# Row sums' constant on GpSimd, reordered first loads, and later weight casts in the head of a window-attention and two-stage MLP kernel

## The chip, the cores and the metric

The kernel runs on one core of one Trainium2 chip. The metric is the device time of one execution in microseconds (us), the median of the runs. A core has five engines that run their own instruction streams and meet only at semaphores: TensorE (PE; its weight loads, PEld, overlap its matmuls), VectorE (DVE), ScalarE (ACT), GpSimd (POOL) and SyncE (SP), which here issues all DMAs. On-chip data lie in SBUF (128 partitions); matmul results land in PSUM banks.

## The reference, cut to what matters

```python
def _attn_ref(q, k, v):            # B=2, H=8, S=576, D=64, window 64
    scores = (1 / np.sqrt(D)) * np.matmul(q, k.transpose(0, 1, 3, 2))
    scores = np.where((rel >= 0) & (rel < window), scores, -1000000000.0)
    scores = scores - np.max(scores, axis=-1, keepdims=True)
    attn = np.exp(scores)
    attn = attn / (np.sum(attn, axis=-1, keepdims=True) + 1e-09)
    return np.matmul(attn, v)
...
    x = attention output as (1152, 512)
    h = x @ w_in; g = np.maximum(h, 0) + np.log1p(np.exp(-np.abs(h)))   # d_ff 2048
    x = g @ w_out
    p = domain_probs / (domain_probs.sum(-1, keepdims=True) + 1e-09)     # 4 experts, 1024 wide
    for e in range(4):
        out += p[:, e:e + 1] * (np.maximum(x @ w1[e], 0) @ w2[e])
```

## The kernel before, in words

Every float32 matmul of the two MLP stages is made of three matmuls on "high" and "low" parts: the high part is the value cast to the engine's rounded float32 type, the low part is what the cast lost. So each weight block is loaded raw, cast (high), and then subtracted (low).

The attention is cut into 24 units of 3 windows of 64 tokens for a pair of heads. Two units share one load of 1 MB (queries and keys, then values), called group 0 to 11. A unit u passes through these steps:

- `scores` on TensorE (line 986), three matmuls into one PSUM bank (`score_bank`); the last raises `score_done`.
- `masked_scores` on VectorE (line 665), mask and row maximum per window.
- `softmax_exp` on ScalarE (line 480), exponential with the row sum of each window; it raises `exp_done`.
- `row_inverse` on VectorE: line 674 adds the reference's 1e-9 (`EPS`) to the 128x3 row sums, and line 676 takes the reciprocal.
- `normalise_first` on VectorE (line 681, three `tensor_scalar`, one per window) for units 0 to 10; later units are normalised on GpSimd by `normalise` (line 422). Both raise `norm_done`.
- `transpose_probs` on TensorE (line 999), `copy_pT` on ScalarE (line 489), `weigh_values` on TensorE (line 1012), then `x_high` on ScalarE (line 496) and `x_low` on VectorE (line 689), which leave the input of the first MLP.

Units 0 to 9 are started ahead of the MLP. From then on a loop over steps k = 0, 1, ... does one 128-wide block of the first MLP a step: the up matmuls (line 1025), then softplus: on ScalarE `absolute` (504), `exponential` (509), `hidden_high` of the step before (521), `logarithm` (516); on VectorE `rounded` (697), `hidden_low` of the step before (716), `relu_ln` (703), `activation` (711); on GpSimd `lost` (429), on which `activation` waits. The down matmuls (1045) come three steps later. The remaining attention units are woven into the same steps: unit k + 10 is scored and exponentiated in step k, unit k + 8 is transposed and weighed. In every step each engine's order is fixed by the order of the calls; an engine waits at the first instruction whose semaphore isn't there, and everything behind it waits too.

The first weight blocks f = 0 to 4 are cast on VectorE (`up_high`, line 847) after the units that `FIRST_SPLIT` names: `{3: 0, 4: 1, 5: 2, 6: 3, 9: 4}`, that is, block 0 after unit 3 and so on. GpSimd subtracts their low parts in halves (`up_low_half`, line 433), ten halves i = 0 to 9. Halves 0 to 3 wait for the cast number i + 1; halves 4 to 9 wait until `norm_done` shows units 7, 8, 8, 9, 9, 9, which keeps them behind VectorE's normalisations. Ahead of half 8 come two halves of the first down block (`down_low_half`, line 440). Only then does GpSimd come to `lost` of step 0.

SyncE issues the loads in the written order on one queue: unit 0's queries and keys in two pieces, those of group 1, values of group 0 and 1, group 2, up weights pair 0, group 3, up weights pair 1, groups 4, 5, 6 (5 and 6 wait for slots), down weights pair 0, up weights pair 2 (which waits for the low parts of blocks 0 and 1, because it overwrites them), the gate's input `probs`, and more.

Of the kernel before, what the change touches and what calls it, by code (L numbers as in the profile page):

```python
# [10 lines left out]
P = 128  # L11
# [43 lines left out]
def two_stage_mlp_after_window_attention(nc, units, w_in, w_out, probs, w1, w2, out):  # L55
    ctx = ExitStack()
    with ctx:
# [152 lines left out]
        def score_bank(u):  # L210
            return ps_score[u % 2 if u < ALT_SCORED else 0]

        def pT_bank(u):
            return ps[3] if u < ALT_UNITS and u % 2 else ps_pT

# [32 lines left out]
        consts = sem("consts")  # L248
        score_done = sem("score_done")
        negmax_done = sem("negmax_done")  # L250
        first_maxima = sem("first_maxima")
        exp_done = sem("exp_done")
        eps_done = sem("eps_done")
        rinv_done = sem("rinv_done")
        norm_done = sem("norm_done")
        pT_done = sem("pT_done")
# [33 lines left out]

        FIRST_SPLIT = {3: 0, 4: 1, 5: 2, 6: 3, 9: 4}
        LATE_SPLIT = {1: 5, 3: 6, 4: 7}

        def f32(ap):
# [12 lines left out]
        def _(sp):  # L309
# [37 lines left out]
            sp.dma_start(slots[0][:, UNIT_QK:2 * UNIT_QK], units[0][:, UNIT_QK:2 * UNIT_QK]).then_inc(scores_landed[0], 16)  # L347
            first_queries_keys(1)
            first_values(0)
            first_values(1)  # L350
            attention_inputs(2)
            up_weights(0, up_in(0), (0,))
            attention_inputs(3)
            up_weights(0, up_in(0), (1,))
            attention_inputs(4)
            attention_inputs(5)
            attention_inputs(6)
            down_weights(0, down_in(0), (0,))
            up_weights(0, up_in(0), (2,))
            sp.dma_start(gate[:, :, :], probs.rearrange("(t p) e -> p t e", p=P)).then_inc(gate_in, 16)  # L360
            down_weights(0, down_in(0), (1,))
            attention_inputs(7)
            up_weights(0, up_in(0), (3,))
# [31 lines left out]
        @block.gpsimd  # L395
        def _(pool):
            steps = [0]

            def step(ins):

                steps[0] += 1
                ins.then_inc(consts, 1)
                pool.wait_ge(consts, steps[0])

            step(pool.memset(mask[:, :, :], 0.0))
            step(pool.memset(ident[:, :], 0.0))

            for h in range(2):
                m = mask[WIN * h:WIN * h + WIN, :, :]
                step(pool.affine_select(out=m, in_=m, compare_op=ALU.is_gt, fill=NEG, base=0,  # L410
                                        pattern=[[0, 2], [1, P]], channel_multiplier=-1))
                step(pool.affine_select(out=m, in_=m, compare_op=ALU.is_ge, fill=NEG, base=WIN,
                                        pattern=[[0, 2], [-1, P]], channel_multiplier=1))
            step(pool.memset(mask[:, 0, 0:WIN], NEG))
            step(pool.affine_select(out=ident[:, :], in_=ident[:, :], compare_op=ALU.not_equal, fill=1.0, base=0,
                                    pattern=[[-1, P]], channel_multiplier=1))
            assert steps[0] == N_CONSTS

            def normalise(u):
                pool.wait_ge(rinv_done, u + 1)  # L420
                p = prob[:, u % 3, :, :]
                pool.tensor_tensor(p, p, rinv[:, u % 3, :].rearrange("p (w o) -> p w o", o=1).to_broadcast([P, 3, P]),
                                   ALU.mult).then_inc(norm_done, 1)

            def lost(n, f):

                s, i = f % 2, h_count(n, f)
                pool.wait_ge(rnd_done, i)
                pool.tensor_tensor(sp_c[:, s, :], sp_e[:, s, :], sp_c[:, s, :], ALU.subtract).then_inc(lost_done, 1)  # L429

            def up_low_half(f, half):
                ks = slice(2 * half, 2 * half + 2)
                low = pool.tensor_tensor(wa[1][:, f, ks, :], raw_a[:, f // 2 % 2, ks, P * (f % 2):P * (f % 2) + P],
                                         f32(wa[0][:, f, ks, :]), ALU.subtract)
                if half == 1:
                    low.then_inc(wa_lo, 1)

            def down_low_half(half):
                cols = slice(DM // 2 * half, DM // 2 * half + DM // 2)
                low = pool.tensor_tensor(wb[1][:, 0, cols], raw_b[:, 0, 0, cols], f32(wb[0][:, 0, cols]), ALU.subtract)  # L440
                if half == 1:
                    low.then_inc(wb_lo, 1)

            for i in range(len(FIRST_SPLIT) - 1):
                pool.wait_ge(wa_hi, i + 1)
                up_low_half(i // 2, i % 2)
            for i, unit in zip(range(len(FIRST_SPLIT) - 1, 2 * len(FIRST_SPLIT)), (7, 8, 8, 9, 9, 9)):
                pool.wait_ge(norm_done, unit + 1)
                if i == 8:
                    pool.wait_ge(wb_hi, 1)  # L450
                    down_low_half(0)
                    down_low_half(1)
                    pool.wait_ge(wa_hi, 5)
                up_low_half(i // 2, i % 2)
            for k in range(STEPS):
                lost(k // FT, k % FT)
                if 0 < k < N_UNITS - SCORED:
                    normalise(k + SCORED)
# [186 lines left out]
        def _(dve):  # L645
# [9 lines left out]

            def masked_scores(u):

                dve.wait_ge(score_done, u + 1)
                if u >= 3:
                    dve.wait_ge(pT_done, u - 2)  # L660
                c, half, _ = unit_place(u)
                first = (2 * c + half) % 3 == 0
                for w in range(3):
                    m = 0 if first and w == 0 else 1
                    e = dve.tensor_tensor_reduce(prob[:, u % 3, w, :], score_bank(u)[:, P * w:P * w + P],
                                                 mask[:, m, :], -SCALE, BIG, ALU.add, ALU.min,
                                                 negmax[:, u % 3, w:w + 1])
                    if u == 0 and w < 2:
                        e.then_inc(first_maxima, 1)
                e.then_inc(negmax_done, 1)  # L670

            def row_inverse(u):
                dve.wait_ge(exp_done, u + 1)
                dve.tensor_scalar(rowsum[:, u % 3, :], rowsum[:, u % 3, :], EPS, None, ALU.add).then_inc(eps_done, 1)
                dve.wait_ge(eps_done, u + 1)
                dve.reciprocal(rinv[:, u % 3, :], rowsum[:, u % 3, :]).then_inc(rinv_done, 1)

            def normalise_first(u):
                dve.wait_ge(rinv_done, u + 1)
                for w in range(3):  # L680
                    m = dve.tensor_scalar(prob[:, u % 3, w, :], prob[:, u % 3, w, :], rinv[:, u % 3, w:w + 1], None,  # L681
                                          ALU.mult)
                m.then_inc(norm_done, 1)

            def x_low(u):
                dve.wait_ge(x_hi, u + 1)
# [287 lines left out]
        def _(pe):  # L974
            def scores(u):
# [7 lines left out]
                if u >= 2:  # L983
                    pe.wait_ge(negmax_done, last_of_score_bank(u))
                for w in range(3):
                    m = pe.matmul(score_bank(u)[:, P * w:P * w + P], q_slots[s][:, u % 2, w, :],  # L986
                                  k_slots[s][:, u % 2, WIN * w:WIN * w + P], start=True, stop=True)
                m.then_inc(score_done, 1)

            def transpose_probs(u):  # L990
# [223 lines left out]
```

## Time and profile before

| | before |
|---|---|
| median of 3 runs | 632.71 us (632.67 to 633.68) |
| the profiled execution, device time | 633.16 us |
| its span in the profile | 631.4 us |
| TensorE busy | 621.4 us, 98% of the span, 3892 matmul instructions |
| VectorE / ScalarE / GpSimd busy | 388.2 / 276.5 / 86.9 us |
| granted TensorE clock | full in all 40 slices |
| DMA | 40.78 MB, mean 65 GB/s; over 400 GB/s for most of the first 25 us |

The profile is one execution recorded by the hardware profiler. Its page gives the busy time of each engine; the chain of waits follows the work back from the last instruction, at each step to what released it; the timeline lists the instructions of an engine in order with the idle time ahead of each and what ended it. Times of rows are in us from the start of the span. Of the 10 us in which TensorE is idle, 5.5 lie before 20.95 us, 1.7 between there and 38 us, and 2.7 in the last 31 us, where the last results are stored; there is next to none between. The change touches the part up to 38 us.

### The profile page before, as it was taken

What the parts mean: (1) busy time and instruction counts of PE and PEld (TensorE: products, weight loads), DVE (VectorE), ACT (ScalarE), POOL (GpSimd) and SP (SyncE); (2) the same over time, 40 slices, a digit from 0 to 9 for tenths busy, and PEclk for the clock granted to TensorE, in tenths of its full rate; (3) what the DMA queues carried; (4) which work ended last, traced back from release to release, by engine and by line L of the source; (5) the groups of instructions that cost most, each with busy time, mean ns of one, the idle gap of its engine ahead of it and who ended that gap; (6) DMA issues with size and microseconds to landing.
All of it is one profiled execution on the core that took longest, in us unless ns stands there. A gap on an engine that the chain in (4) does not pass through costs nothing.

```text
span 631.4 us, 10158 instructions
## 1 busy us (share of the span) xinstructions
PE 621.4 (98%) x3892; PEld 578.6 (92%) x3892; DVE 388.2 (61%) x869; ACT 276.5 (44%) x635; POOL 86.9 (14%) x85
## 2 busy tenths in 40 slices
PE   7989999999999999999999999999999999999998
PEld 6789999999999999998998998988988988988987
DVE  5887665568645588897267267277276276376342
ACT  5887755556544465552342342332332332432410
POOL 1453333333333332000000000000000000000000
PEclk9999999999999999999999999999999999999999
DMA  8905230033200010022103003003003004000012
GB/s 326 375 36 194 75 134 1 19 115 134 67 2 0 2 33 28 7 68 94 42 0 101 34 1 100 34 1 104 31 1 113 21 1 123 12 0 1 2 51 100
DMA packets 11728, 40.78 MB, mean 65 GB/s; under 512 B 2336, under 2 KB 2592, under 8 KB 10400
## 3 DMA queue, kind: packets, MB, share of 16 engines
q1 hardware_dynamic: 11680, 40.13, 18.0%
q8 instruction: 31, 0.51, 0.3%
q14 instruction: 17, 0.14, 0.1%
HBM read 37.77 MB, written 2.36 MB: 64 GB/s over the span
## 4 chain that ended last, share of the span: by engine, by line
PE 95%; DMA 2%; SPq 1%; ACT 1%; DVE 0%; issue 0%
PE banks L1100 31%; PE banks L1076 28%; PE banks L1025 16%; PE banks L1045 16%; DMA part<-in_units 2%; PE banks L986 2%; PE banks L1012 1%; PE banks L999 1%; PE banks L1092 0%; SPq L315 0%; SPq L331 0%; DVE prob L681 0%; ACT prob L480 0%; SPq L323 0%; ACT sp_e L509 0%
## 5 line engine op out<-in xcount | busy, mean ns | idle before, releaser
L1100 PE MATMUL banks<-wb_hi,ehid_hi 128*128 128x512 f32 x284 | 110.5, 389 | 0.0
L1100 PE MATMUL banks<-wb_lo,ehid_hi 128*128 128x512 f32 x284 | 110.5, 389 | 0.0
L1100 PE MATMUL banks<-wb_hi,ehid_lo 128*128 128x512 f32 x284 | 110.5, 389 | 0.0
L429 POOL TENSOR_TENSOR sp_c<-sp_e,sp_c 128x384 f32<-128x384 f32 x48 | 64.1, 1336 | 135.5 <-DVE sp_c L697 135.5
L839 DVE SCALAR_TENSOR_TENSOR part<-banks,gate,part 128x512 f32<-128x512 f32 x62 | 46.6, 751 | 54.0 <-PE banks L1100 54.0
L1076 PE MATMUL banks<-T_lo,aop_hi 128*128 128x288 f32 x256 | 75.6, 295 | 0.0
L1076 PE MATMUL banks<-T_hi,aop_lo 128*128 128x288 f32 x256 | 75.6, 295 | 0.0
L1076 PE MATMUL banks<-T_hi,aop_hi 128*128 128x288 f32 x256 | 75.3, 294 | 0.0
L1025 PE MATMUL banks<-xy_hi,wa_hi 128*128 128x384 f32 x192 | 66.2, 345 | 0.0
L1045 PE MATMUL banks<-hid_hi,wb_hi 128*128 128x384 f32 x192 | 65.8, 343 | 0.0
L1045 PE MATMUL banks<-hid_hi,wb_lo 128*128 128x384 f32 x192 | 64.3, 335 | 0.0
L1045 PE MATMUL banks<-hid_lo,wb_hi 128*128 128x384 f32 x192 | 64.3, 335 | 0.0
L1025 PE MATMUL banks<-xy_hi,wa_lo 128*128 128x384 f32 x192 | 64.2, 335 | 0.0
L1025 PE MATMUL banks<-xy_lo,wa_hi 128*128 128x384 f32 x192 | 64.2, 334 | 0.0
L1100 PEld LDWEIGHTS banks<-wb_hi,ehid_lo 128*128 128x128 f32 x284 | 53.3, 188 | 11.1
L1100 PEld LDWEIGHTS banks<-wb_hi,ehid_hi 128*128 128x128 f32 x284 | 53.3, 188 | 10.8
L1100 PEld LDWEIGHTS banks<-wb_lo,ehid_hi 128*128 128x128 f32 x284 | 53.3, 188 | 10.7
L504 ACT ACTIVATE sp_e<-banks 128x384 f32<-128x384 f32 x48 | 23.5, 490 | 76.0 <-PE banks L1025 76.0
L1076 PE MATMUL banks<-B_hi,aop_lo 128*128 128x288 f32 x192 | 56.7, 295 | 0.0
L1076 PE MATMUL banks<-B_lo,aop_hi 128*128 128x288 f32 x192 | 56.6, 295 | 0.0
L1076 PE MATMUL banks<-B_hi,aop_hi 128*128 128x288 f32 x192 | 56.4, 294 | 0.0
L552 ACT ACTIVATE kept<-banks 128x576 f32<-128x576 f32 x16 | 10.4, 650 | 90.9 <-PE banks L1076 90.9
(105 smaller groups left out, 1245.6 us busy)
## 6 DMA issues: line engine op xcount, KB each, us to landing
unit_in<-in_units SPq DMA_DIRECT2D x8, 1024.0 KB, 6.7
raw_a<-in_w SPq DMA_DIRECT2D x16, 512.0 KB, 3.3
raw_b<-in_w SPq DMA_DIRECT2D x16, 512.0 KB, 3.3
raw_a<-in_w_in SPq DMA_DIRECT2D x8, 512.0 KB, 5.3
raw_b<-in_w_out SPq DMA_DIRECT2D x8, 512.0 KB, 4.1
part<-in_units SPq DMA_DIRECT2D x2, 1024.0 KB, 13.4
out_dram<-part SPq DMA_DIRECT2D x8, 256.0 KB, 2.0
unit_in<-in_units SPq DMA_DIRECT2D x2, 384.0 KB, 7.2
```

Of the source, the lines that this page charges most:

```text
L429: pool.tensor_tensor(sp_c[:, s, :], sp_e[:, s, :], sp_c[:, s, :], ALU.subtract).then_inc(lost_done, 1)
L504: act.activation(sp_e[:, s, :], up_bank(i - 1)[:, 0:CH], ACT.Abs).then_inc(abs_done, 1)
L552: act.activation(kept[i][:, :, :], Z[i], ACT.Copy).then_inc(p1_copied, 1)
L839: dve.scalar_tensor_tensor(out=acc[:, T, :], in0=TOKEN_BANKS[T], scalar=gate[:, T, e:e + 1], in1=acc[:, T, :], op0=ALU.mult, op1=ALU.add). ...
L986: m = pe.matmul(score_bank(u)[:, P * w:P * w + P], q_slots[s][:, u % 2, w, :], k_slots[s][:, u % 2, WIN * w:WIN * w + P], start=True, stop ...
L999: m = pe.transpose(pT_bank(u)[:, P * w:P * w + P], prob[:, u % 3, w, :], ident[:, :])
L1012: m = pe.matmul(o_bank(u)[D * h:D * h + D, WIN * w:WIN * w + WIN], v_slots[s][:, w, c:c + D], probT[:, u % 2, w, WIN * h:WIN * h + WIN], s ...
L1025: m = pe.matmul(bank[:, 0:CH], wa[a][:, f, k, :], xy[x][:, c, k, :], start=(k == 0 and i == 0), stop=(k == KT - 1 and i == 2))
L1045: m = pe.matmul(sums[t][:, 0:CH], wb[a][:, f, P * t:P * t + P], hid[x][:, f, :], start=(f == 0 and i == 0), stop=(f == FT - 1 and i == 2))
L1076: m = pe.matmul(into[:, s, :], aop[a][:, i, row, k, :], bop[name][b][:, k, HC * s:HC * s + HC], start=(fresh and k == 0 and j == 0), stop= ...
L1100: m = pe.matmul(TOKEN_BANKS[T], ehid[x][:, i, P * T:P * T + P], wb[a][:, f, :], start=(i == 0 and j == 0), stop=(i == 3 and j == 2))
```

## The change

It makes five edits.

1. The load order: group 2 ahead of group 1's values, group 3 ahead of up weights pair 0. `probs` is laid out on the host so that each partition's 36 values are one run of 144 bytes instead of nine of 16.
2. The casts: block 0 after unit 4 instead of 3, and so on up to block 3 after unit 7; block 4 stays after unit 9.
3. For units 2 to 9 the addition of `EPS` moves from VectorE to GpSimd (`add_eps`): units 2, 3, 4 ahead of half 0, then one ahead of each of halves 0 to 3 (units 5 to 8), and that of unit 9 ahead of half 5. Each waits for `exp_done` of its unit.
4. `normalise_first` becomes one `tensor_tensor` of 128x384 against the broadcast reciprocals, for units 0 to 10.
5. The three score matmuls of unit 0 go to three banks, each with its own signal, so that the mask and maximum of a window start before the other two are done.

```diff
+        def score_block(u, w):
+            bank = (score_bank(0), ps[1], ps[2])[w] if u == 0 else score_bank(u)
+            return bank[:, P * w:P * w + P]
...
-        FIRST_SPLIT = {3: 0, 4: 1, 5: 2, 6: 3, 9: 4}
+        FIRST_SPLIT = {4: 0, 5: 1, 6: 2, 7: 3, 9: 4}
+        EPS_AHEAD = range(2, SCORED)
...
             first_values(0)
+            attention_inputs(2)
             first_values(1)
-            attention_inputs(2)
+            attention_inputs(3)
             up_weights(0, up_in(0), (0,))
-            attention_inputs(3)
             up_weights(0, up_in(0), (1,))
...
-            sp.dma_start(gate[:, :, :], probs.rearrange("(t p) e -> p t e", p=P)).then_inc(gate_in, 16)
+            sp.dma_start(gate[:, :, :], probs).then_inc(gate_in, 16)
...
+            def add_eps(u):
+                pool.wait_ge(exp_done, u + 1)
+                pool.tensor_scalar(rowsum[:, u % 3, :], rowsum[:, u % 3, :], EPS, None, ALU.add).then_inc(eps_ahead, 1)
+
+            add_eps(2)
+            add_eps(3)
+            add_eps(4)
             for i in range(len(FIRST_SPLIT) - 1):
+                add_eps(5 + i)
                 pool.wait_ge(wa_hi, i + 1)
                 up_low_half(i // 2, i % 2)
             for i, unit in zip(range(len(FIRST_SPLIT) - 1, 2 * len(FIRST_SPLIT)), (7, 8, 8, 9, 9, 9)):
+                if i == 5:
+                    add_eps(unit + 1)
                 pool.wait_ge(norm_done, unit + 1)
...
-                dve.wait_ge(score_done, u + 1)
+                if u > 0:
+                    dve.wait_ge(score_done, u + 1)
...
+                    if u == 0 and w < 2:
+                        dve.wait_ge(first_scores, w + 1)
+                    elif u == 0:
+                        dve.wait_ge(score_done, 1)
...
-                dve.tensor_scalar(rowsum[:, u % 3, :], rowsum[:, u % 3, :], EPS, None, ALU.add).then_inc(eps_done, 1)
-                dve.wait_ge(eps_done, u + 1)
+                if u not in EPS_AHEAD:
+                    dve.tensor_scalar(rowsum[:, u % 3, :], rowsum[:, u % 3, :], EPS, None,
+                                      ALU.add).then_inc(eps_done, 1)
+                if u in EPS_AHEAD:
+                    dve.wait_ge(eps_ahead, u - EPS_AHEAD[0] + 1)
+                else:
+                    dve.wait_ge(eps_done, u + 1 if u < EPS_AHEAD[0] else u + 1 - len(EPS_AHEAD))
                 dve.reciprocal(rinv[:, u % 3, :], rowsum[:, u % 3, :]).then_inc(rinv_done, 1)
...
-                for w in range(3):
-                    m = dve.tensor_scalar(prob[:, u % 3, w, :], prob[:, u % 3, w, :], rinv[:, u % 3, w:w + 1], None,
-                                          ALU.mult)
-                m.then_inc(norm_done, 1)
+                p = prob[:, u % 3, :, :]
+                dve.tensor_tensor(p, p, rinv[:, u % 3, :].rearrange("p (w o) -> p w o", o=1).to_broadcast([P, 3, P]),
+                                  ALU.mult).then_inc(norm_done, 1)
```

## Rows read from the trace of the kernel before

**Rows 1.** The page: busy time of TensorE, share of the span, instructions
```profile
PE 621.4 (98%) x3892; PEld 578.6 (92%) x3892; DVE 388.2 (61%) x869; ACT 276.5 (44%) x635; POOL 86.9 (14%) x85
```

**Rows 2.** Chain of waits, first 90 us: start, duration, what the end waited for
```profile
5.83 15.08 DMA part<-in_units
...
37.27 0.45 issue
```

**Rows 3.** Timeline of TensorE, first 40 us: start, duration, instruction, idle before
```profile
8.09 0.94 PE L986 MATMUL banks<-unit_in 128*128 128x128 f32 x6 [1.99 <-DMA unit_in<-in_units]
...
26.17 0.44 PE L1025 MATMUL banks<-xy_hi,wa_hi 128*128 128x384 f32 x1
...
33.97 0.55 PE L999 MATMUL banks<-ident,prob 128*128 128x128 f32 x3 [1.06 <-DVE prob L681]
```

**Rows 4.** Timeline of GpSimd, first 45 us
```profile
3.64 0.15 POOL L414 MEMSET mask<- 128x64 f32 x1
...
26.42 1.43 POOL L433 TENSOR_TENSOR wa_lo<-raw_a,wa_hi 128x256 fp32r<-128x256 f32 x2 [1.17 <-DVE prob L681]
28.96 0.84 POOL L433 TENSOR_TENSOR wa_lo<-raw_a,wa_hi 128x256 fp32r<-128x256 f32 x1 [1.12 <-DVE prob L681]
29.77 1.54 POOL L440 TENSOR_TENSOR wb_lo<-raw_b,wb_hi 128x256 fp32r<-128x256 f32 x2
31.27 1.41 POOL L433 TENSOR_TENSOR wa_lo<-raw_a,wa_hi 128x256 fp32r<-128x256 f32 x2
32.64 0.99 POOL L429 TENSOR_TENSOR sp_c<-sp_e,sp_c 128x384 f32<-128x384 f32 x1
...
37.22 1.07 POOL L422 TENSOR_TENSOR prob<-prob,rinv 128x384 f32<-128x384 f32 x1 [0.59 <-DVE rinv L676]
```

**Rows 5.** Timeline of VectorE, first 40 us
```profile
27.79 0.17 DVE L674 TENSOR_SCALAR rowsum<-rowsum 128x3 f32<-128x3 f32 x1 [0.79 <-ACT prob L480]
...
28.20 0.68 DVE L681 TENSOR_SCALAR prob<-prob,rinv 128x128 f32<-128x128 f32 x3
28.80 0.42 DVE L847 CAST wa_hi<-raw_a 128x512 fp32r<-128x512 f32 x1
29.56 0.29 DVE L665 CUSTOM_DVE_ANT_0 prob<-banks,mask 128x128 f32<-128x128 f32 x1 [0.34 <-PE banks L986]
...
30.20 0.52 DVE L697 TENSOR_SCALAR sp_c<-sp_e 128x384 f32<-128x384 f32 x1
...
32.31 1.60 DVE L681 TENSOR_SCALAR prob<-prob,rinv 128x128 f32<-128x128 f32 x3
33.83 0.55 DVE L711 TENSOR_TENSOR sp_l<-sp_l,sp_c 128x384 f32<-128x384 f32 x1
...
34.93 0.35 DVE L697 TENSOR_SCALAR sp_c<-sp_e 128x384 f32<-128x384 f32 x1
...
37.05 0.55 DVE L711 TENSOR_TENSOR sp_l<-sp_l,sp_c 128x384 f32<-128x384 f32 x1
37.51 1.32 DVE L648 TENSOR_TENSOR wa_lo<-raw_a,wa_hi 128x512 fp32r<-128x512 f32 x1
```

**Rows 6.** Instructions of line 648: count, then shortest, median and longest in ns
```profile
L648 DVE TENSOR_TENSOR wa_lo<-raw_a,wa_hi x11: 676/684/1319, 37.5 to 148.8; 128x512 fp32r<-128x512 f32 x11
```

**Rows 7.** Timeline of ScalarE, first 40 us
```profile
24.35 0.19 ACT L480 ACTIVATION_READ_ACCUMULATOR prob<-prob,negmax 128x1 f32 x1
...
27.57 0.19 ACT L480 ACTIVATION_READ_ACCUMULATOR prob<-prob,negmax 128x1 f32 x1
...
34.41 0.53 ACT L521 ACTIVATE hid_hi<-sp_l 128x384 fp32r<-128x384 f32 x1 [1.25 <-DVE sp_l L711]
...
37.14 0.47 ACT L489 ACTIVATE probT<-banks 128x384 f32<-128x384 f32 x1
```

**Rows 8.** SyncE's queue: the issue of up weights pair 2
```profile
23.45 0.33 SPq L331 DMA_DIRECT2D raw_a<-in_w_in  x1
```

**Rows 9.** Its time from issue to landing, us
```profile
DMA to landing us min/median/max: 4.9/4.9/4.9
```

More of the change, by code:

```diff
@@ L250, in two_stage_mlp_after_window_attention @@
         negmax_done = sem("negmax_done")
+        first_scores = sem("first_scores")
         first_maxima = sem("first_maxima")
@@ L253, in two_stage_mlp_after_window_attention @@
         eps_done = sem("eps_done")
+        eps_ahead = sem("eps_ahead")
         rinv_done = sem("rinv_done")
@@ L664, in masked_scores @@
                     m = 0 if first and w == 0 else 1
-                    e = dve.tensor_tensor_reduce(prob[:, u % 3, w, :], score_bank(u)[:, P * w:P * w + P],
+                    if u == 0 and w < 2:
+                        dve.wait_ge(first_scores, w + 1)
+                    elif u == 0:
+                        dve.wait_ge(score_done, 1)
+                    e = dve.tensor_tensor_reduce(prob[:, u % 3, w, :], score_block(u, w),
                                                  mask[:, m, :], -SCALE, BIG, ALU.add, ALU.min,
@@ L985, in scores @@
                 for w in range(3):
-                    m = pe.matmul(score_bank(u)[:, P * w:P * w + P], q_slots[s][:, u % 2, w, :],
+                    m = pe.matmul(score_block(u, w), q_slots[s][:, u % 2, w, :],
                                   k_slots[s][:, u % 2, WIN * w:WIN * w + P], start=True, stop=True)
+                    if u == 0 and w < 2:
+                        m.then_inc(first_scores, 1)
                 m.then_inc(score_done, 1)
@@ L1199 @@
         "w_out": inputs["moe_w_out"].reshape(FF1 // 256, 2, P, DM).transpose(0, 2, 1, 3),
-        "probs": inputs["moe2_domain_probs"],
+        "probs": inputs["moe2_domain_probs"].reshape(N_TOK, P, NE).transpose(1, 0, 2),
         "w1": np.stack([w1[:, 0, :, :, 0], w1[:, 1, :, :, 0], w1[:, 1, :, :, 1], w1[:, 0, :, :, 1]]).transpose(
```

## The prediction

> **What bounds the kernel now.** I read the page first: TensorE is busy 621.4 of 631.4 us [rows 1], so a change outside its work can only move the 10 us in which it idles. The chain of waits then shows where these lie. Its first long piece is the transfer of group 4, issued at 5.83 and landed 15.08 later, at 20.91 [rows 2]; the scores of unit 8 start on it at 20.95. Behind that the chain is TensorE with two real stalls: 1.06 us ahead of the transpose of unit 10 at 33.97 [rows 3], and 0.45 us ahead of the value matmuls of unit 10, W10 for short, which start at 37.27 + 0.45 = 37.72 [rows 2]. From W10 on the chain has no further gap up to 90 us. So two clocks count: when group 4 lands, and when W10 may start. Whatever the change does between is worth what it moves W10, and nothing more.
>
> What W10 waits for is read backwards. Its input is copied by ScalarE at 37.14 [rows 7]. ScalarE's order in step 1 is hidden_high, logarithm, x_high, exponentials of unit 11, a weight cast, then that copy; it runs through these without a pause from 34.41, where it had idled 1.25 us for VectorE's `activation` of step 0 [rows 7]. That one started at 33.83 [rows 5]. It needs two things: VectorE must be through the normalisation of unit 10 (three instructions, 32.31, 1.60 us) [rows 5], and GpSimd's `lost` of step 0 must be done: 32.64 + 0.99 = 33.63 [rows 4]. They came within 0.2 us of each other. So W10 starts 37.72 - 33.83 = 3.89 us after `activation`, and the change has to be judged by the later of these two.
>
> **Load order, gate, late casts: nothing, with cover.** The bytes ahead of group 4 are the same and it is still issued last of them, so I keep 20.91; groups 2 and 3 land earlier and the work behind them then waits longer for group 4. Bounds: if the order of packets changes how evenly the engines drain, some tenths of a us either way; I take 0. The first scores of unit 0 in three banks: the next thing TensorE does, scores of unit 2, waits for a transfer until 8.09, 1.99 us idle [rows 3], and an earlier softmax of unit 0 ends inside that wait. 0. The casts one unit later, and `add_eps` of unit 8 ahead of half 3, hold up the low part of block 1. That addition can't start before the exponentials of unit 8 end at 24.35 + 0.19 = 24.54 [rows 7]; add about 0.15 and a half of about 0.7, and the low part stands at 25.45. TensorE wants it at 26.17 [rows 3]: 0.7 us of cover. SyncE's load of up weights pair 2, which waited for the same low part and was issued at 23.45 [rows 8], moves to about 25.5, with the gate, down weights pair 1 and group 7 behind it. It landed 4.9 us after its issue [rows 9], behind a full queue; with the same 4.9 it lands at 30.4, with a shorter queue nearer 29. The cast that needs it comes at about 29.5 in the sum below, so it costs 0 to 0.9 us on VectorE, whose next steps have some slack. I take 0.
>
> **The transpose of unit 10: a gain that is not kept.** The three `tensor_scalar` of unit 10 took 1.60 us where unit 9's took 0.68 [rows 5], because the second lay under GpSimd's `lost`. One `tensor_tensor` of 384 columns takes 0.46 us to the next instruction (37.05 to 37.51) [rows 5]. Started at 32.31, or a little later, it lets the transpose run at about 32.9 to 33.4: 0.6 to 1.06 us earlier. But TensorE then only reaches W10's wait earlier.
>
> **GpSimd's `lost` of step 0: the term that decides.** Before, halves 5 and 6 ran at 26.42 to 27.85, in a time when GpSimd would otherwise wait, and half 7 began at 28.96, behind the normalisation of unit 9 [rows 4]. Now `add_eps` of unit 9 stands ahead of half 5, and waits for the exponentials of unit 9, which end at 27.57 + 0.19 = 27.76 [rows 7]; these hang on TensorE's order behind group 4 and don't move. Seven pieces (halves 5, 6, 7, two down halves, 8, 9) then stand between 27.76 and `lost`, instead of five from 28.96.
>
> 1. The addition: the trace has no such instruction on GpSimd. A memset of 64 columns took 0.15 [rows 4], a half of 256 columns 0.7; three columns lie nearest to the memset. With 0.08 us until GpSimd sees the signal (the normalisation ended at 28.88, half 7 began at 28.96 [rows 4, 5]) half 5 starts at about 27.95; bounds 27.8 and 28.5.
> 2. Seven pieces at 31.27 to 32.64 for two, 0.69 each [rows 4]: 4.83 us.
> 3. What VectorE takes from them. The rows show that the two engines don't run side by side in these operations. `split_up` of 512 columns took 1.32 us at 37.51, under GpSimd's normalisation 37.22 to 38.29 [rows 4, 5], where its median is 0.684 [rows 6]; so it began to work at 38.15, 0.14 before GpSimd's recorded end. `rounded` took 0.52 at 30.20 instead of 0.35 at 34.93 [rows 5], and the two down halves around it 1.54 instead of 1.41 [rows 4]: 0.13 for a `tensor_scalar` of 384 columns. Half 7 took 0.84 for 0.72 (1.43 for two at 26.42), its start lying 0.16 into the cast at 28.80 [rows 4, 5]: 0.12, and 0.2 if the two had met squarely. Four such meetings now lie in GpSimd's run: the normalisation of unit 9 (wanted at about 28.2, in the middle of half 5; a `tensor_tensor` with both inputs in SBUF, 0.46 less the 0.14 of overlap: 0.33), the cast of block 4 (behind half 6, 0.2), `rounded` (0.13 to 0.2), the normalisation of unit 10 (0.33). Sum 1.0; bounds 0 and the full lengths of the four, 0.46 + 0.33 + 0.27 + 0.46 = 1.5.
>
> `lost` then starts at 27.95 + 4.83 + 1.0 = 33.8, ends at 34.8, and `activation` starts at about 34.9 instead of 33.83: 1.1 later. ScalarE's row of step 1 follows at once, and W10 starts at 38.8. ScalarE's other waits in that row (maxima of unit 11) hang on the same VectorE order and move with it. TensorE has no idle time behind W10 from which to make this good.
>
> The Trainium skill ("SBUF — State Buffer", Who interferes with whom) says that VectorE with two SBUF inputs and GpSimd share a port pair by an exclusive lock: the one that issues first keeps it for the whole instruction. The trace agrees in kind (1.32 for 0.684 us) [rows 5, 6], but VectorE got in 0.14 us before the recorded end. Taken to the letter, the rule gives the upper bound of item 3.
>
> **The sum.** Span 631.4 + 1.1 = 632.5 us, device time of the profiled execution 633.16 + 1.1 = 634.3. That execution was 0.45 above the median of the runs, so against 632.71 I say 633.8 us, 0.17% longer. A difference under about 0.2%, 1.27 us, is what a measurement of this kernel can't tell from none. So the forecast is "same", close to its upper edge.
>
> **The rivals.**
> A. The forecast, W10 later by 0.8 to 1.4 us: 0.47, of which 0.13 over 1.27.
> B. VectorE and GpSimd hardly hinder each other here, because the `tensor_tensor` fits between GpSimd's accesses: only the late start of half 5 counts, 27.95 + 4.83 + 0.99 = 33.8 for the end of `lost`, W10 later by 0 to 0.8, time 632.7 to 633.5, middle 632.9. For it: `activation` at 37.05 kept its 0.55 although GpSimd began at 37.22 [rows 4, 5]. Against: GpSimd's instruction then took 1.07. 0.20.
> C. Slower: each meeting costs GpSimd the whole VectorE instruction, and after each both want the port at once. The place is 28.2 to 33.2; `lost` ends at 27.98 + 4.9 + 1.5 + 0.99 = 35.4, W10 is 1.6 later, 634.3. It decides from the point at which the four meetings cost over 1.2 us together, or the addition over 0.35 us instead of 0.15. With a small GpSimd instruction of 0.5 us it is 634.7. 0.24.
> D. Group 4 lands at another time, since the transfers ahead of it are reordered. For a result faster than 631.44 it must land 2.4 us earlier, or 1.3 if the rest stays as before. The same bytes stand ahead of it, issued by the same time, which speaks against. Earlier enough 0.05, later enough 0.04.
> That the change does what it is shaped for, all the 1.06 us of unit 10 kept, would need `lost` done by about 32.8; GpSimd alone forbids it (item 2 with nothing for item 3 already ends at 33.8), so it has no chance of its own.
>
> **How the numbers follow.** Faster is the early half of D: 0.05. Slower is 0.13 of A, C and the late part of D: 0.41. Same is the rest of A and B: 0.54. The range runs from inside B to C with a dearer addition: 632.5 to 635.0; outside remain D early and the ends of B and C, under 0.2.
>
> **What would show it.** In the changed profile: scores of unit 8 at 20.9 still, with some 1.5 us of idle ahead of it instead of a few tenths; half 5 at about 28.0, right behind a short addition; the normalisations of units 9 and 10 longer than 0.55 us; the transpose of unit 10 near 33.3; `lost` at 33.8; `activation` right behind its end; the wait ahead of W10 grown from 0.45 to about 2.2 us. The forecast is wrong if half 5 starts before 27.8, if `lost` starts before 33.2 or after 34.5, if ScalarE's hidden_high isn't released by `activation`, or if unit 8's scores leave 20.9 by more than 0.3.

## The result and the profile after

| | before | after |
|---|---|---|
| median | 632.89 us (632.67 to 633.68, 6 runs) | 635.84 us (634.64 to 636.99, 6 runs) |
| ratio | | 1.0046, 95% interval 1.0036 to 1.0056 |
| profiled execution, its span | 633.16, 631.4 us | 635.89, 634.1 us |
| mean granted TensorE clock | 1.00 | 0.997 (0.994 in two other runs) |

The change costs 2.95 us, 0.46%. The forecast was 633.8 us, 0.17%, with a range up to 635.0: too little. In the profiled executions all of the loss lies ahead of W10, the value matmuls of unit 10, as in the forecast: behind W10 both spans have 593.7 us left (631.4 - 37.72 and 634.1 - 40.43). Of all the executions below one, of b3 (682.5 us, mean clock 0.852), was over 1.5% above the fastest of its kernel; it counts in that run's median and in no ratio, share or other count.

TensorE's timeline after the change, first 45 us: start, duration, instruction, idle time before it. Line 1012 are scores, 1027 transposes, 1040 value matmuls.

```profile
7.69 0.94 PE L1012 MATMUL banks<-unit_in 128*128 128x128 f32 x6 [1.09 <-DMA unit_in<-in_units]
...
21.05 0.94 PE L1012 MATMUL banks<-part 128*128 128x128 f32 x6 [2.42 <-DMA part<-in_units]
...
23.85 1.48 PE L1012 MATMUL banks<-part 128*128 128x128 f32 x6
25.27 0.91 PE L1040 MATMUL banks<-probT,part 128*64 128x64 f32 x12
...
27.28 0.57 PE L1040 MATMUL banks<-probT,part 128*64 128x64 f32 x12
...
35.70 0.55 PE L1027 MATMUL banks<-ident,prob 128*128 128x128 f32 x3 [0.96 <-DVE prob L708]
...
40.43 0.57 PE L1040 MATMUL banks<-probT,unit_in 128*64 128x64 f32 x12 [1.41 <-issue]
```

The same groups before (line 986 are scores, 999 transposes, 1012 value matmuls):

```profile
20.02 0.55 PE L999 MATMUL banks<-ident,prob 128*128 128x128 f32 x3 [0.34 <-DVE prob L681]
20.95 0.94 PE L986 MATMUL banks<-part 128*128 128x128 f32 x6 [0.39 <-DMA part<-in_units]
...
25.67 0.57 PE L1012 MATMUL banks<-probT,part 128*64 128x64 f32 x12
...
37.72 0.57 PE L1012 MATMUL banks<-probT,unit_in 128*64 128x64 f32 x12 [0.45 <-issue]
```

Group 4 landed where it did (scores of unit 8 at 21.05, before 20.95), but TensorE had idled 2.42 us for it instead of 0.39. The scores of unit 9 then took 1.48 us and the value matmuls of unit 6 0.91, where such groups otherwise take 0.83 and 0.57. The windows say why. Columns: stretch, its length, busy time of TensorE, its weight loads, VectorE, ScalarE, GpSimd, then the granted clock, DMA share, GB/s:

```profile
18.65:21.05 2.40, 0.01 (x1) 0.01 (x1) 1.59 (x8) 1.64 (x7) 1.33 (x4) 1.00 0.99 396
21.05:22.50 1.45, 1.45 (x19) 1.26 (x20) 0.48 (x5) 0.00 (x0) 0.36 (x1) 1.00 1.00 412
22.50:26.00 3.50, 3.50 (x24) 3.26 (x24) 2.12 (x13) 1.97 (x8) 1.07 (x3) 0.53 0.74 303
26.00:28.00 2.00, 1.90 (x23) 1.44 (x20) 1.27 (x6) 0.94 (x3) 0.57 (x1) 0.98 0.44 147
```

Behind the idle stretch the granted clock is at half, the lower of its two levels (1.2 instead of 2.4 GHz), for 3.4 us (from 22.7 to 26.1); before the change it stayed at 1.00 here. TensorE is what everything hangs on in this stretch, so the slow clock goes straight into the time: from the scores of unit 8 to the value matmuls of unit 7 it is 27.28 - 21.05 = 6.23 us, before 25.67 - 20.95 = 4.72. That is 1.51 us. From there to W10 it is 13.15 us, before 12.05: 1.10 us. With 0.10 for the landing these make 2.71, the difference of the profiled executions (635.89 - 633.16 = 2.73).

The second term is the one that was forecast. GpSimd after the change (line 453 is `add_eps`, 440 and 447 the halves, 436 `lost`), to be read beside [rows 4]:

```profile
24.85 0.23 POOL L453 TENSOR_SCALAR rowsum<-rowsum 128x3 f32<-128x3 f32 x1 [3.44 <-ACT prob L497]
25.16 1.41 POOL L440 TENSOR_TENSOR wa_lo<-raw_a,wa_hi 128x256 fp32r<-128x256 f32 x2
29.45 0.23 POOL L453 TENSOR_SCALAR rowsum<-rowsum 128x3 f32<-128x3 f32 x1 [2.88 <-ACT prob L497]
29.75 2.61 POOL L440 TENSOR_TENSOR wa_lo<-raw_a,wa_hi 128x256 fp32r<-128x256 f32 x3
32.32 1.53 POOL L447 TENSOR_TENSOR wb_lo<-raw_b,wb_hi 128x256 fp32r<-128x256 f32 x2
33.82 1.41 POOL L440 TENSOR_TENSOR wa_lo<-raw_a,wa_hi 128x256 fp32r<-128x256 f32 x2
35.20 1.31 POOL L436 TENSOR_TENSOR sp_c<-sp_e,sp_c 128x384 f32<-128x384 f32 x1
```

And VectorE, to be read beside [rows 5] (708 normalisation, 873 cast, 723 `rounded`, 729 `relu_ln`, 697 the addition of unit 10, 737 `activation`):

```profile
29.99 0.91 DVE L708 TENSOR_TENSOR prob<-prob,rinv 128x384 f32<-128x384 f32 x1
30.82 0.95 DVE L873 CAST wa_hi<-raw_a 128x512 fp32r<-128x512 f32 x1
...
32.32 0.95 DVE L723 TENSOR_SCALAR sp_c<-sp_e 128x384 f32<-128x384 f32 x1
33.19 0.54 DVE L729 SCALAR_TENSOR_TENSOR sp_l<-banks,sp_l 128x384 f32<-128x384 f32 x1
...
33.92 0.65 DVE L697 TENSOR_SCALAR rowsum<-rowsum 128x3 f32<-128x3 f32 x1
...
34.82 0.83 DVE L708 TENSOR_TENSOR prob<-prob,rinv 128x384 f32<-128x384 f32 x1
36.54 0.56 DVE L737 TENSOR_TENSOR sp_l<-sp_l,sp_c 128x384 f32<-128x384 f32 x1 [0.89 <-POOL sp_c L436]
```

The addition on GpSimd waits 2.88 us for the exponentials of unit 9. Seven pieces follow without a pause. The normalisations, the cast, `rounded` and the small addition of unit 10 on VectorE, which meet them, take 1.5 to 4 times their time (0.91 and 0.83 for 0.56, 0.95 for 0.42, 0.95 for 0.35, 0.65 for 0.17). `relu_ln`, which reads PSUM, keeps its 0.54 (0.55 at 40.12 before). `activation` waits 0.89 us for `lost`, and W10 comes 40.43 - 36.54 = 3.89 us behind `activation`, exactly as before.

### The profile page after: what moved, and what is told of

It is laid out like the page before. It is cut to its first block, busy times and chain, and to the rows that moved or that the text cites. A ratio compares the mean times of both kernels' runs of the same rounds, so it can differ in the third digit from the quotient of the medians.

```text
span 634.1 us, 10144 instructions
## 1 busy us (share of the span) xinstructions
PE 623.3 (98%) x3892; PEld 580.5 (92%) x3892; DVE 387.4 (61%) x839; ACT 276.7 (44%) x635; POOL 89.3 (14%) x93
## 4 chain that ended last, share of the span: by engine, by line
PE 95%; DMA 2%; DVE 1%; SPq 1%; issue 1%; ACT 0%; POOL 0%; DVEq 0%
PE banks L1128 30%; PE banks L1104 28%; PE banks L1073 16%; PE banks L1053 16%; DMA part<-in_units 2%; PE banks L1012 2%; PE banks L1040 1%; PE banks L1027 1%; PE banks L1120 0%; ACT prob L497 0%; SPq L322 0%; SPq L338 0%; SPq L330 0%; DVE wa_hi L873 0%; DVE prob L708 0%
## 6 DMA issues: line engine op xcount, KB each, us to landing
part<-in_units SPq DMA_DIRECT2D x2, 1024.0 KB, 13.1
```

## The experiments

There are two suspects: the clock (TensorE idle ahead of group 4, 1.5 us) and GpSimd's `lost` (1.1 us). Since a single execution either has a stretch at half clock or not, each run is also read by how many of its executions have a mean granted clock of 0.997 or less. One half-clock stretch of 3.4 us makes 0.997 of 634 us, two make 0.995. After the change this was so in 6 of 6, and in the kernel before, in the runs beside the experiments, in 10 of 99.

The ratio is close to that of the mean times, so it gives a few long times more weight than the median does (a4 above all). The kernel before was run again beside each set: its medians were 632.96 us for the runs a, 632.89 for the runs b, 632.74 for the runs c.

| run | ratio to before | median us | executions with a clock of 0.997 or less |
|---|---|---|---|
| a1 fill | 1.0029 (1.0019 to 1.0038) | 634.74 | 4 of 10 |
| a2 unit 9 | 1.0005 (0.9989 to 1.0021) | 633.08 | 6 of 10 |
| a3 both | 1.0002 (0.9993 to 1.0012) | 633.19 | 0 of 10 |
| a4 old load order | 1.0024 (1.0004 to 1.0044) | 633.68 | 4 of 10 |
| c1 old load order, unit 9 | 0.9991 (0.9981 to 1.0000) | 632.20 | 1 of 10 |
| b1 loads and casts on before | 1.0009 (0.9999 to 1.0020) | 633.76 | 6 of 10 |
| b2 GpSimd late on before | 1.0019 (1.0010 to 1.0029) | 633.96 | 2 of 10 |
| c4 normalisation on before | 0.9998 (0.9989 to 1.0007) | 632.85 | 3 of 10 |
| b3 two fills, unit 9 | 0.9996 (0.9987 to 1.0005) | 633.11 | 0 of 9 |
| b4 `lost` first on before | 0.9990 (0.9981 to 0.9999) | 632.17 | 1 of 11 |
| c2 the same, blocks spread | 0.9980 (0.9971 to 0.9989) | 631.87 | 1 of 11 |
| c3 b3 and c2 together | 0.9986 (0.9977 to 0.9995) | 631.91 | 2 of 12 |

**a1, the idle stretch filled.** On the changed kernel:

```diff
+            for _ in range(8):
+                pe.matmul(ps[0][:, 0:P], warm[:, :], warm[:, :], start=True, stop=True)
             scores(UPC)
```

> The changed kernel with eight matmuls on the zeroed warm-up tile (results unused, bank ps[0]) between the transpose of unit 5 and the scores of unit 8, so that TensorE works through most of the 2.42 us in which it was idle. Theory 1 (clock: the idle stretch ahead of group 4's landing lets the granted clock fall to half from 22.5 to 26.1, worth 1.6 us; GpSimd's late lost of step 0 the other 1.1): granted clock 1.00 throughout, transpose of unit 7 at 24.5 to 24.7, W10 at 38.7 to 38.9, about 1.6 us under the changed kernel and 1.1 over the kernel before. Rival (the clock falls for a reason that isn't the idle stretch, as the chip's state): granted clock 0.5 there as before, time unchanged.

In the profiled execution the clock stayed at 1.00, and W10 came 38.30 - 20.33 = 17.97 us after the scores of unit 8, 1.2 over the 16.77 of before: the half-clock term is gone, the GpSimd term stands. The median fell by 1.1 us, not 1.6, because 4 of 10 executions still had a slow stretch (635.1 to 636.0 us); the six at full clock have a median of 633.97, 1.0 over before. None of the four has a profile, so the place of their stretch wasn't seen; a4 below suggests where.

**a2, the addition of unit 9 back on VectorE.**

```diff
-        EPS_AHEAD = range(2, SCORED)
+        EPS_AHEAD = range(2, SCORED - 1)
...
-                if i == 5:
-                    add_eps(unit + 1)
```

> The changed kernel with unit 9's addition back on VectorE, so that half 5 on GpSimd no longer waits for unit 9's exponentials. Theory 1: the clock still falls (idle 2.4 us ahead of unit 8's scores), halves 5 and 6 run right behind half 4, lost of step 0 starts 1.0 to 1.4 us earlier than the 35.20 of the changed kernel, W10 about 1.0 earlier, 1.6 to 1.9 us over the kernel before. Rival (GpSimd's order doesn't matter, all is the clock): lost moves but W10 doesn't, time as the changed kernel.

It gained more than expected, 2.8 us on the changed kernel's 635.84. In the profile W10 is 37.70 - 20.59 = 17.11 us after unit 8's scores, against 17.97 in a1, so the addition's place was worth 0.9. The rest is the spread of the clock: 6 of 10 executions have it under 1 (633.0 to 635.9 us), the four others lie at 631.8 to 632.0, under the kernel before. In this profile the half clock lies at another place, behind the wait for group 1. The windows of TensorE alone (length, busy time, granted clock, DMA share, GB/s):

```profile
6.50:8.60 2.10, 0.00 (x1) 1.00 1.03 421
8.60:12.10 3.50, 3.50 (x17) 0.53 1.02 425
12.10:14.00 1.90, 1.90 (x29) 0.97 0.98 410
```

There it cost nothing ahead of group 4, since TensorE still had to wait for it afterwards (0.20 us, until 20.59). So what a slow stretch costs depends on what comes behind it.

**a3, both edits.**

> Both edits together: filling matmuls and unit 9's addition on VectorE. Theory 1: both losses gone, within 0.4 us of the kernel before (the remaining difference is unit 10's transpose, earlier by 0.6 to 1.0, which ends in the wait of W10). If the two terms don't add up to all of the loss, it stays over 1 us above.

As expected: within 0.3 us of before, and no execution of ten with a slow clock, against 6 of 10 in a2, whose only difference is the eight matmuls. This pair, with b3 below (0 of 9), carries the claim that idle time is what lets the clock fall here. It doesn't say where: a2's one profiled fall lay behind the wait for group 1, which a3 leaves unfilled (1.03 us there in its profile). And the filling saved next to no time: a3's median of 633.19 us isn't under a2's 633.08. The filling was too long for the best executions: unit 8's scores began at 20.24 straight behind it, without a wait for the transfer.

**a4, the load order of before in the changed kernel.**

> The changed kernel with the load order of before (group 1's values ahead of group 2, up weights pair 0 ahead of group 3); casts, additions and normalisation as changed. Theory 1: groups 2 and 3 land about 1 us later, the idle stretch ahead of unit 8's scores shrinks to 1.0 to 1.5 us; if the clock then holds, 1.6 us under the changed kernel, if it still falls, the faster VectorE row is a cause beside the load order. Rival (the order of packets itself slows things): group 4 would land at another time than 20.9 to 21.0.

TensorE idled 1.50 us ahead of unit 8's scores (group 4 landed at 21.56 here), and the clock held there. It fell elsewhere, behind the wait ahead of W10:

```profile
39.54 0.57 PE L1040 MATMUL banks<-probT,unit_in 128*64 128x64 f32 x12 [2.13 <-issue]
```

```profile
37.40:39.54 2.14, 0.01 (x2) 1.00 0.00 0
39.54:40.10 0.56, 0.56 (x13) 0.99 0.00 0
40.10:43.40 3.30, 3.30 (x12) 0.50 0.00 0
43.40:45.00 1.60, 1.60 (x14) 0.97 0.00 0
```

(First fence: TensorE's timeline; second: its windows.) The landing at 21.56 is the sign that I gave for the rival, but the other profiles show landings as far apart with either load order (see rival D below), so it doesn't speak for it. The fall ahead of W10's row I had not foreseen: where the transpose of unit 10 comes early, GpSimd's lateness gathers in one long wait ahead of W10, and this can cost a slow stretch too, 1.5 us: 634.7 - 39.54 = 595.2 us are left behind W10 instead of 593.7. Five of the six executions at full clock took 632.7 to 632.9 us, no more than before, although GpSimd is as late here as in the changed kernel; more on that under c1.

**c1, the load order of before and unit 9's addition on VectorE.**

> The changed kernel with the load order of before and unit 9's addition on VectorE; the one difference from the run with the load order of before is that GpSimd's lost of step 0 comes earlier, so that TensorE idles about 1.4 instead of 2.13 us ahead of W10. Theory 1 (the half clock seen from 40 us in that run follows the long idle stretch ahead of W10): no fall behind W10, fewer executions with a clock under 1 than 4 of 10, median 632.0 to 632.6. Rival (falls come from the head alone): as many executions under 1.

1 of 10 executions with a slow clock instead of 4 of 10, and 632.20 us, 0.5 under the 632.74 of before beside it, with an interval that reaches 1. The profiled execution happened to be the one with a fall. It began 0.7 us behind the end of a stretch of 1.43 us idle ahead of unit 8, so a fall in the head doesn't need the new load order.

With a2 it separates the loads: the same kernel with the new load order has 6 of 10. Ten executions each are few, and all runs together are firmer: with the new load order and no filling 18 of 26 executions had a slow clock (after, a2, b1), with the old one 22 of 161 (before, a4, b2, b4, c1, c2, c4). The late casts are in 20 of the latter (a4, c1), with 5.

At full clock the rest of the change does gain. a2's four such executions (631.8 to 632.0 us) and c1's nine (632.1 to 632.8) are under before, and five of a4's six aren't above it in spite of GpSimd. No such execution of these three has a profile, so where they gain wasn't seen. A reading that fits, and isn't shown: TensorE is ready for group 4 earlier than before (end of unit 5's transpose at 18.6 us in the changed kernel, 19.3 in c1, 20.6 before), which is worth something whenever group 4 lands early.

**b1, load order and late casts alone, on the kernel before.** The edit is the two diffs of the change on `attention_inputs(2)`, `attention_inputs(3)` and `FIRST_SPLIT`.

> The kernel before with two parts of the change alone: groups 2 and 3 loaded ahead, and the casts of blocks 0 to 3 one unit later. Additions and normalisation stay on VectorE as before. Theory 1 (the clock falls where TensorE idles about 2 us): VectorE still holds unit 5 to 7 back, so the idle stretch ahead of unit 8's scores is 1 to 1.6 us; clock 1.00 in most executions, time within 0.5 us of before, W10 16.8 after unit 8's scores as before. Rival (the new load order is what makes executions spread): median over 1 us above before with clocks under 1.

The rival came nearer to the truth: 6 of 10 executions with a slow clock. In the profile the idle stretch ahead of unit 8's scores was 1.03 us, 0.34 us of idle lay a little ahead of it, and the clock fell 0.35 us after the scores had begun:

```profile
18.57 0.55 PE L999 MATMUL banks<-ident,prob 128*128 128x128 f32 x3 [0.34 <-DVE prob L681]
20.14 1.35 PE L986 MATMUL banks<-part 128*128 128x128 f32 x6 [1.03 <-DMA part<-in_units]
```

```profile
19.10:20.14 1.04, 0.01 (x1) 1.00 0.97 394
20.14:23.50 3.36, 3.35 (x23) 0.55 1.02 417
```

So the falls come without the moved additions and the single normalisation, and 2 us of idle time aren't needed. That it is the load order and not the late casts, which b1 has too, is said by a4 and c1 (5 of 20 with the casts late and the old order). W10 was 38.41 - 20.14 = 18.27 us after unit 8's scores, 1.50 over before, the price of one stretch once more.

**b2, GpSimd's halves 5 and 6 late, on the kernel before.**

```diff
-            for i, unit in zip(range(len(FIRST_SPLIT) - 1, 2 * len(FIRST_SPLIT)), (7, 8, 8, 9, 9, 9)):
+            for i, unit in zip(range(len(FIRST_SPLIT) - 1, 2 * len(FIRST_SPLIT)), (7, 9, 9, 9, 9, 9)):
```

> The kernel before with one edit: halves 5 and 6 on GpSimd wait for the normalisation of unit 9 instead of unit 8, so that seven pieces stand between 28.9 and lost of step 0, with no other part of the change. Theory 1: lost starts at 34.0 instead of 32.64, W10 1.2 to 1.4 later, time 1.2 to 1.4 us over before; transposes up to unit 10 where they were. If the idle stretch ahead of W10 reaches 2 us the clock may fall behind it in some executions, another 1.5. Rival (GpSimd's order has slack): time as before.

The executions with full clock lie at 633.7 to 634.7, their middle at 633.9, 1.0 over before (1.1 over its executions at full clock). The GpSimd term is thus shown alone, on the old kernel, with no other part of the change. The profiled execution is one of the two with a fall, which came 0.5 us after the scores of unit 8 had begun, with the old load order and an idle stretch of 1.07 us:

```profile
21.03 1.19 PE L986 MATMUL banks<-part 128*128 128x128 f32 x6 [1.07 <-DMA part<-in_units]
```

```profile
30.53 2.35 POOL L433 TENSOR_TENSOR wa_lo<-raw_a,wa_hi 128x256 fp32r<-128x256 f32 x3 [5.48 <-DVE prob L681]
32.84 1.42 POOL L440 TENSOR_TENSOR wb_lo<-raw_b,wb_hi 128x256 fp32r<-128x256 f32 x2
34.22 1.41 POOL L433 TENSOR_TENSOR wa_lo<-raw_a,wa_hi 128x256 fp32r<-128x256 f32 x2
35.58 1.01 POOL L429 TENSOR_TENSOR sp_c<-sp_e,sp_c 128x384 f32<-128x384 f32 x1
```

From the value matmuls of unit 7, behind the fall, to W10 it is 40.52 - 27.25 = 13.27 us, 1.2 over the 12.05 of before.

**c4, the normalisation by one instruction alone, on the kernel before.**

> The kernel before with the normalisation of units 0 to 10 by one tensor_tensor and nothing else of the change. Theory 1 (a gain that isn't kept): VectorE 0.13 us a unit faster up to unit 9, transpose of unit 10 at 33.2 to 33.4 instead of 33.97, but W10 where it was within 0.2 us, since lost of step 0 and ScalarE's row set it; time within 0.3 us of before; the idle stretch ahead of W10 grows from 0.45 to about 1.1. Rival: the transpose's 0.7 us is kept, time 0.6 us under before.

No gain, as expected, but for another reason than I gave. The transpose of unit 10 wasn't earlier at all (13.1 us after unit 8's scores, before 13.0), for the single instruction waited behind `lost` as the three had. VectorE (674 the addition, 681 the normalisation), then GpSimd:

```profile
31.72 0.75 DVE L674 TENSOR_SCALAR rowsum<-rowsum 128x3 f32<-128x3 f32 x1 [0.53 <-ACT prob L480]
32.50 0.18 DVE L676 RECIPROCAL rinv<-rowsum 128x3 f32<-128x3 f32 x1
32.71 1.10 DVE L681 TENSOR_TENSOR prob<-prob,rinv 128x384 f32<-128x384 f32 x1
```

```profile
32.39 1.00 POOL L429 TENSOR_TENSOR sp_c<-sp_e,sp_c 128x384 f32<-128x384 f32 x1
```

0.68 of the 1.10 us lie under `lost` (32.71 to 33.39). The idle stretch ahead of W10 didn't grow either (0.44 us instead of the 1.1 expected).

**b3, two shorter fills.** On a2: three filling matmuls ahead of `scores(2)`, four ahead of `scores(UPC)`, the scores of unit 8.

> The changed kernel with unit 9's addition on VectorE and filling matmuls in two places, three ahead of the scores of unit 2 and four ahead of those of unit 8 (results unused). Theory 1: neither idle stretch reaches 2 us, clock 1.00 in nearly all executions, and with only four instead of eight filling matmuls the scores of unit 8 start as soon as group 4 lands: median 632.0 to 632.8, spread under 1.5 us. Rival (clock falls without an idle stretch of that length): executions with a clock under 1 stay as many as without the fills (6 of 10).

No execution of nine had a slow clock (one at 0.999). The median (633.08 of these nine) missed the expectation by 0.3: the executions fall into two lots, 631.8 to 632.2 and 633.1 to 633.8, between which the clock doesn't differ. In the profiled one, of the lower lot, group 4's scores start at 19.71. I take the landing of group 4 to be the cause, but the upper lot has no profile, so this stays open.

**b4 and c2, `lost` ahead of the last halves, on the kernel before.** c2 in full (b4 has `{2: 5, 3: 6, 4: 7}`):

```diff
-        LATE_SPLIT = {1: 5, 3: 6, 4: 7}
+        LATE_SPLIT = {2: 5, 4: 6, 5: 7}
...
                     down_low_half(1)
+                    lost(0, 0)
+                    pool.wait_ge(norm_done, SCORED + 1)
                     pool.wait_ge(wa_hi, 5)
...
-                lost(k // FT, k % FT)
+                if k > 0:
+                    lost(k // FT, k % FT)
...
             def normalise_first(u):
                 dve.wait_ge(rinv_done, u + 1)
+                if u == SCORED:
+                    p = prob[:, u % 3, :, :]
+                    dve.tensor_tensor(p, p, rinv[:, u % 3, :].rearrange("p (w o) -> p w o", o=1).to_broadcast([P, 3, P]),
+                                      ALU.mult).then_inc(norm_done, 1)
+                    return
```

> The kernel before with lost of step 0 ahead of halves 8 and 9 on GpSimd (these wait for the normalisation of unit 10), unit 10 normalised by one tensor_tensor, and ScalarE's and VectorE's share of weight block 5 moved one step later. Theory 1 (W10 hangs on lost and on ScalarE's row behind it): transpose of unit 10 at 32.9, activation of step 0 at 32.8, W10 at 36.2 instead of 37.7, time 1.0 to 1.5 us under before (631.4 to 631.9). Rival (another wait takes its place, as the weight block moved later or halves 8 and 9): gain under 0.4 us.

> As the run with lost of step 0 ahead of halves 8 and 9, but with weight blocks 5, 6, 7 in steps 2, 4 and 5, so that VectorE has the low part of the second down block in time (TensorE had waited 0.53 us for it at 46.25). Theory 1: that wait is gone, W10 as in that run 15.7 us after the scores of unit 8, time 1.0 to 1.3 us under before (631.6 to 631.9). Rival (another wait comes in its place): no gain over that run's 632.17.

b4 gained 0.7 us, less than expected: the wait ahead of W10 was gone, but another took its place in step 4, where TensorE waited for the second down block (W10 itself at 35.95, forecast 36.2):

```profile
46.25 0.41 PE L1053 MATMUL banks<-hid_hi,wb_hi 128*128 128x384 f32 x1 [0.53 <-DVE wb_lo L656]
```

c2 spreads the weight blocks, and this wait is gone too. W10 is at 35.94, 15.76 us after unit 8's scores (20.18) instead of 16.77; `lost` starts at 30.82:

```profile
30.82 1.00 POOL L429 TENSOR_TENSOR sp_c<-sp_e,sp_c 128x384 f32<-128x384 f32 x1
32.73 1.89 POOL L433 TENSOR_TENSOR wa_lo<-raw_a,wa_hi 128x256 fp32r<-128x256 f32 x2 [0.91 <-DVE prob L685]
```

(The expectation says that this distance was 15.7 in b4 too; there it was 35.95 - 19.70 = 16.25.) At 631.87 us, 0.2% under before with the interval clear of 1, c2 beats both kernels. It is the same step that the change made worse, turned the other way.

**c3, everything together.**

> The changed kernel with unit 9's addition on VectorE, filling matmuls (three ahead of the scores of unit 2, four ahead of those of unit 8), lost of step 0 ahead of halves 8 and 9, and weight blocks 5, 6, 7 in steps 2, 4 and 5. Theory 1 (the change's head is sound once TensorE doesn't idle long and GpSimd isn't late): clock 1.00 in nearly all executions, W10 15.6 us after the scores of unit 8, median 631.0 to 631.8, the fastest of all. Rival: what the head gains is lost at group 4's landing, so it equals the kernel before with the later two edits.

It has the fastest single execution (630.73), but its median of 631.91 is 0.1 over the expected range and no better than c2's, so the expectation of the fastest of all is missed. 2 of 12 still had a slow clock. The profiled execution is one of them: group 4's scores began at 20.72, 1.0 us later than in b3, TensorE idled 1.58 us in spite of the four matmuls, and the half clock followed from 22.2 to 25.6.

## Why the prediction was wrong

- **What bounds the kernel.** Right. In both profiles the span is W10's start plus 593.7 us, and the two clocks named, group 4's landing and W10, are the right ones.
- **"Load order, gate, late casts: nothing, with cover."** This is the step that failed. The landing was as said (21.05 for 20.9) and no transfer came too late. But I wrote that the work behind groups 2 and 3 "then waits longer for group 4" as if waiting were free. The wait was forecast as 1.5 us and was 2.42 (transpose of unit 5 at 18.08 instead of 20.02). Counted from the scores of unit 2, that transpose came 11.93 us later before, 10.82 in b1 with the loads and casts alone, 10.39 after the change: most of it comes with the loads and casts, the rest with VectorE's shorter row. Behind it the granted clock fell to half for 3.4 us, which cost 1.5 us and stands in the sum as nothing. Only the trace of before stood at my hand, with a clock of 1.00 in all slices, even behind 1.99 us of idle at 8.09 [rows 3]; from that I took it that the clock wasn't in play, and gave it neither a rival nor a price. a3 against a2 shows that it hangs on the idle time, and c1 against a2, with the counts of all runs, that the new load order makes it frequent. The old order has it too, in 22 of 161 executions.
- **The transpose of unit 10.** Forecast 0.6 to 1.06 us earlier, and ending in the wait of W10. In the changed kernel it wasn't: 35.70 - 21.05, less the 1.51 of the slow clock, is 13.14 us after unit 8's scores, before 13.02. So the wait ahead of W10 was 1.41 us and not 2.2. The addition of unit 10 took 0.65 us and the normalisation 0.83, both beside GpSimd. In c4, without the rest, it wasn't earlier either: the instruction took 1.10 us. The cost of 0.46 that I took for it is that of an instruction that meets no GpSimd work. In a1 and a2, where it didn't lie under `lost`, it did come earlier (12.4 to 12.6 us after unit 8's scores instead of 13.0), and W10 took nothing from it, as said.
- **GpSimd's `lost`.** Right in mechanism and size. From the end of unit 9's exponentials (29.36) it is 0.39 us to half 5 (forecast 0.19; the addition is 0.23 long, and 0.3 from start to start), 5.84 to the start of `lost` (forecast 6.0) and 7.15 to its end (forecast 7.0). W10 was 1.10 us later on this account (forecast 1.1), in b2 and a1 1.2. In the times of executions at full clock the term is 1.1 (b2 over before) and 0.8 (a1 over a3, a4 over c1). `lost` started at 35.20, past the 34.5 that I named as a sign of being wrong, but that is the slow clock ahead of it: from the exponentials on, it was in time.
- **Rival C,** every meeting at full length, gave 1.6 us. The Trainium skill's rule of the exclusive lock ("SBUF — State Buffer", Who interferes with whom) holds in kind: cast 0.95 for 0.42, `rounded` 0.95 for 0.35, both under GpSimd's pieces. But over the seven pieces GpSimd lost 0.62 us (29.75 to 35.20 is 5.45, seven at 0.69 are 4.83), and in `lost`, which the normalisation of unit 10 met, 0.32 (1.31 for 0.99). Together that is 0.94 us, near the 1.0 of the forecast and under the 1.5 of the rival.
- **Rival D,** another landing of group 4. By the start of unit 8's scores it had landed at 19.7 us or before (b3) to 21.05 with the new load order, and at 19.7 or before (b4) to 21.56 (a4) with the old one; I had allowed some tenths. Between the two profiled executions it makes 0.10 us, but it is a spread of nearly 2 us that the single profile of before (20.91) hid.
- **The range.** With 1.1 us from GpSimd and 1.5 from the clock the sum would have been 635.3 to 635.5, on a median of before of 632.71 or 632.89. Two of the six executions after the change (636.8 and 637.0 us) have a mean clock of 0.994, so they had more than one such stretch.

## What to carry to other kernels

Making work ready earlier ahead of a transfer that sets the pace can lose: the bounding engine idles in one piece instead of several, and its clock may fall just when the transfer lands and the critical row begins. Price a longer idle stretch of TensorE by what the half clock costs in the row behind it. Letting it multiply zeros took the falls away where nothing else was late (6 of 10 to 0 of 10), but in a3 it gained no time. c2, which shortens the wait on GpSimd instead, came 0.2% under before with no filling. And an instruction that moves to another engine brings its wait along: what counts is not its 0.23 us but the two halves of 0.7 us queued behind it, that had been done for free.

## What the runs showed of the hardware that I had not expected

- The granted clock fell to half behind idle stretches of 2.42 (after), 2.11 (a2), 2.13 (a4), 1.58 (c3), 1.43 (c1), 1.07 (b2) and 1.03 us (b1), each time for 3.4 us, beginning 0.2 (a2) to 1.6 us (after) after work had begun again. It did not fall behind others of 1.99 (before), 2.12 (a1), 1.50 (a4), 1.44 (b2, ahead of W10) and 1.22 us (c4). The same kernel can have it in one execution and not in the next. One profile with a full clock therefore proves little; here the share of executions told more.
- A stretch at half clock cost 1.5 us where TensorE was the bound, and nothing where a transfer bound it afterwards (a2).
- An addition of three columns on VectorE, 0.17 us alone, took 0.65 and 0.75 us beside a running GpSimd instruction: small `tensor_scalar` instructions wait for it as large ones do. The reciprocal of the same three columns right behind kept its 0.17 and 0.18.
